# Later batches' queries transposed by VectorE in 32 by 32 blocks instead of by TensorE

## What is computed

```
q_s = exp(q - max over features); q_s /= sum over features + 1e-9
k_s = exp(k - max over tokens);   k_s /= sum over tokens + 1e-9
x = q_s @ (k_s^T @ v)                      per batch and head -> [4608, 512]
x = relu(x @ w_in)^2 @ w_out               512 -> 2048 -> 512
x = (silu(xn @ w_gate) * (xn @ w_val)) @ moe2_w_out,  xn = x / rms(x) * rms_g   512 -> 1536 -> 512
```

## Time and profile before

| | |
|---|---|
| median of 3 runs | 1659.6 us (1659.34 to 1660.26) |
| the profiled execution, its own time | 1660.84 us |
| its span in the trace | 1659.1 us |
| TensorE busy | 1642.0 us, 99% |
| VectorE, ScalarE, GpSimd busy | 1155.2, 616.8, 595.6 us |
| granted TensorE clock over the span | 0.999 of full speed |

### The profile page before, as it was taken

One profiled execution on the slowest core, in us unless ns is written; L12 is line 12 of the kernel. 1 busy time (PEld: TensorE's weight loads), 2 busy tenths in 40 slices (PEclk: granted clock), 3 DMA queues, 4 the chain that ended last, 5 costly groups with the idle time before them and its releaser, 6 DMA issues.

```text
span 1659.1 us, 27077 instructions
## 1 busy us (share of the span) xinstructions
PE 1642.0 (99%) x10246; PEld 1494.9 (90%) x10246; DVE 1155.2 (70%) x1752; ACT 616.8 (37%) x1056; POOL 595.6 (36%) x469
## 2 busy tenths in 40 slices
PE   7999999999999999999999999999999999999999
PEld 6999999999988888888888988988998989999999
DVE  6687667666667778888766565546555568877785
ACT  5544334333323333333334333323333334434442
POOL 4554324332102225342237644556455553000000
PEclk9999999999999999999999999999999999999999
DMA  7675545554653453444341323232321335443441
GB/s 260 200 247 182 172 163 184 185 175 134 213 176 84 127 172 115 123 122 124 109 158 71 105 93 112 87 127 89 108 88 65 112 124 178 153 153 121 147 140 52
DMA packets 151745, 230.10 MB, mean 139 GB/s; under 512 B 11840, under 2 KB 75840, under 8 KB 151616
## 3 DMA queue, kind: packets, MB, share of 16 engines
q1 hardware_dynamic: 151616, 228.38, 42.4%
HBM read 143.39 MB, written 84.93 MB: 138 GB/s over the span
## 4 chain that ended last, share of the span: by engine, by line
PE 93%; DVE 2%; POOL 2%; issue 1%; ACT 1%; SPq 0%; DMA 0%; DVEq 0%; ACTq 0%; POOLq 0%
PE bank L1882 16%; PE bank L1884 16%; PE bank L1883 16%; PE bank L1968 7%; PE bank L1969 7%; PE bank L1970 7%; PE bank L2057 5%; PE bank L2059 5%; PE bank L2058 5%; PE bank L1875 2%; PE bank L1855 1%; PE bank L1871 1%; PE bank L1903 1%; PE bank L1904 1%; PE bank L1905 1%
## 5 line engine op out<-in xcount | busy, mean ns | idle before, releaser
L1882 PE MATMUL bank<-TR,SW 128*128 128x512 f32 (+1 forms) x840 | 308.7, 367 | 0.3 <-DVE TR L1590 0.3
L1884 PE MATMUL bank<-TR,SW 128*128 128x512 f32 (+1 forms) x840 | 308.7, 368 | 0.0
L1883 PE MATMUL bank<-TR,SW 128*128 128x512 f32 (+1 forms) x840 | 308.6, 367 | 0.0
L1882 PE MATMUL bank<-TAR,SA 128*128 128x288 f32 x784 | 249.0, 318 | 0.1
L1883 PE MATMUL bank<-TAR,SA 128*128 128x288 f32 x784 | 231.2, 295 | 0.0
L1884 PE MATMUL bank<-TAR,SA 128*128 128x288 f32 x784 | 230.4, 294 | 0.0
L1968 PE MATMUL bank<-GH,W 128*128 128x512 f32 x576 | 224.2, 389 | 0.4 <-DVE GH L1495 0.4
L1969 PE MATMUL bank<-GH,W 128*128 128x512 f32 x576 | 224.2, 389 | 0.0
L1970 PE MATMUL bank<-GH,W 128*128 128x512 f32 x576 | 224.2, 389 | 0.0
L1172 ACT ACTIVATE GH<-g 128x512 fp32r<-128x512 f32 x144 | 91.1, 633 | 241.6 <-DVE g L1490 161.4
L2058 PE MATMUL bank<-SW,OA 128*128 128x256 f32 x630 | 178.3, 283 | 0.0
(11 more groups left out here) (178 smaller groups left out, 3306.0 us busy)
## 6 DMA issues: line engine op xcount, KB each, us to landing
h_scratch<-hb SPq DMA_DIRECT2D x128, 288.0 KB, 2.6
hst<-h_scratch SPq DMA_DIRECT2D x144, 256.0 KB, 2.7
araw<-a_scratch SPq DMA_DIRECT2D x18, 1536.0 KB, 6.8
a_scratch<-group SPq DMA_DIRECT2D x72, 256.0 KB, 2.0
xst<-xn_scratch SPq DMA_DIRECT2D x10, 1024.0 KB, 5.4
xn_scratch<-x SPq DMA_DIRECT2D x9, 1024.0 KB, 5.4
a_scratch<-group SPq DMA_DIRECT2D x48, 192.0 KB, 1.9
out<-ost SPq DMA_DIRECT2D x36, 256.0 KB, 2.0
```

Source lines behind the costliest of these rows:

```text
L1882: nc.tensor.matmul(ps[:, 0:w], w_hi[:, cc], x_hi[:, c], start=opens and c == 0, stop=False, skip_group_check=True)
L1883: nc.tensor.matmul(ps[:, 0:w], w_lo[:, cc], x_hi[:, c], start=False, stop=False, skip_group_check=True)
L1884: last = nc.tensor.matmul(ps[:, 0:w], w_hi[:, cc], x_lo[:, c], start=False, stop=c == 1, skip_group_check=True)
```

## The change

For batches 1 to 7 the host lays out the queries so that a partition holds (head, half of the features, token within a block of 32), and its row holds 18 token blocks by 32 features. A transpose of each 32 by 32 block within its 32 partitions then gives qT. Because a token's 64 features are now on two groups of 32 partitions, maxima and sums are taken over 32 features and combined: ScalarE copies each quarter's column to the neighbouring quarter (four small copies, twice per unit), and VectorE takes the maximum or the sum of both. The rounds Q0 and Q1 and their reads are gone for the later batches; one VectorE transpose (qturn) takes their place, and X0 and X1 wait for it. There is one DMA for q instead of two. Batch 0 is as before.

```diff
-UNIT_PE = [("KM", -3), ("Q0", 0), ("Q1", 1), ("KV", 2), ("X0", 6), ("X1", 7)]
-UNIT_DVE = [("qmax", -10), ("qsum", -6), ("qinv", -6), ("kmax", -9), ("readKM", -2), ("readKV", 3)]
-UNIT_ACT = [("qexp", -7), ("kexp", -1), ("readQ0", 1), ("readQ1", 2), ("readX0", 7), ("readX1", 8)]
-UNIT_POOL = [("qsub", -9), ("qnorm", -4)]
+UNIT_PE = [("KM", -3), ("KV", 2), ("X0", 6), ("X1", 7)]
+UNIT_DVE = [("qmax", -12), ("kmax", -9), ("qmax2", -9), ("qsum", -6), ("qinv", -3), ("readKM", -2), ("qturn", 0), ("readKV", 3)]
+UNIT_ACT = [("qmaxswap", -10), ("qexp", -7), ("qsumswap", -4), ("kexp", -1), ("readX0", 7), ("readX1", 8)]
+UNIT_POOL = [("qsub", -9), ("qnorm", -3)]
...
-            qn[i], at = place(f"qn{i}", at, [P, SJ, 2, D])
+            qn[i], at = place(f"qn{i}", at, [P, SB, DQ])
...
-        CONSTS, CONSTS_ALONE, CONSTS_Q = 13, 6, 2
+        CONSTS, CONSTS_ALONE, CONSTS_Q = 11, 6, 2
...
+        def swap_quarters(dst, src):
+
+            for i in range(P // DQ):
+                rows, other = slice(i * DQ, (i + 1) * DQ), slice((i ^ 1) * DQ, (i ^ 1) * DQ + DQ)
+                last = nc.scalar.activation(dst[rows, :], src[other, :], ACT.Copy)
+            return last
...
-                if unit(b, c) > KC + 2:
-                    sp.wait_ge(rnd_ready, ROUND_NO[b - (c < 2), "Q1", (c - 2) % KC])
+                if b:
+                    if unit(b, c) > KC + 2:
+                        sp.wait_ge(q_turn, unit(b, c) - KC - 2)
+                    sp.dma_start(bufs(b, c).q, qb_d[b - 1, c]).then_inc(loads(b, c)[1][0], 16)
+                    return
...
-                lambda: nc.gpsimd.memset(qn[0][TAIL:P, FULL], 0.0),
-                lambda: nc.gpsimd.memset(qn[1][TAIL:P, FULL], 0.0),
...
+                if b and what == "qsub":
+                    pool.wait_ge(q_max2, u - KC)
+                    nc.gpsimd.tensor_tensor(q, q, over_block(qmax_own[:, :]), ALU.subtract).then_inc(q_sub, 1)
+                    return
+                if b:
+                    pool.wait_ge(q_inv, u)
+                    nc.gpsimd.tensor_tensor(q, q, over_block(qscale[:, :]), ALU.mult).then_inc(q_norm, 1)
+                    return
...
+                elif what == "qmaxswap":
+                    act.wait_ge(q_max, u)
+                    swap_quarters(qmax_other, qmax_own).then_inc(q_maxswap, 1)
+                elif what == "qsumswap":
+                    act.wait_ge(q_sum, u)
+                    swap_quarters(qsum_other, qsum_own).then_inc(q_sumswap, 1)
...
+                elif what == "qmax2":
+                    dve.wait_ge(q_maxswap, u - KC)
+                    nc.vector.tensor_tensor(qmax_own[:, :], qmax_own[:, :], qmax_other[:, :], ALU.max).then_inc(q_max2, 1)
...
+                elif what == "qturn":
+                    dve.wait_ge(q_norm, u)
+                    if (b, c) != (1, 0):
+                        dve.wait_ge(rnd_ready, ROUND_NO[b - (c < 1), "X1", (c - 1) % KC])
+                    nc.vector.transpose(m.qT, m.q.rearrange("p n d -> p (n d)")).then_inc(q_turn, 1)
+                elif what == "qinv" and b:
+                    dve.wait_ge(q_sumswap, u - KC)
+                    nc.vector.scalar_tensor_tensor(qsum_own[:, :], qsum_own[:, :], EPS_SUM, qsum_other[:, :], ALU.add, ALU.add)\
+                      .then_inc(q_den, 1)
+                    dve.wait_ge(q_den, u)
+                    dve.wait_ge(q_norm, u - 1)
+                    nc.vector.reciprocal(qscale[:, :], qsum_own[:, :]).then_inc(q_inv, 1)
...
-                    wait_taken(pe, ROUND_NO[b, "Q1" if half else "Q0", c] - 1)
+                    if b:
+                        pe.wait_ge(q_turn, u - KC)
+                    else:
+                        wait_taken(pe, ROUND_NO[b, "Q1" if half else "Q0", c] - 1)
...
+    qb = q[1:].reshape(B - 1, KC, 2, SB, DQ, 2, DQ).transpose(0, 1, 2, 5, 4, 3, 6).reshape(B - 1, KC, P, SB, DQ)
```

More of the change, by code:

```diff
@@ L20 @@
 TA = S // 2
+DQ = 32
+SB = S // DQ
 FA, FB = 2048, 1536
@@ L310, with build @@
 Bufs = namedtuple("Bufs", "kT q v ekS qT bd kmax qmax")
-def build(nc, q4_d, q1_d, kT_d, k5_d, v4_d, v1_d, w1_d, s1_d, w2_d, wB_d, gv_d, out):
+def build(nc, q4_d, q1_d, qb_d, kT_d, k5_d, v4_d, v1_d, w1_d, s1_d, w2_d, wB_d, gv_d, out):
     h_d = nc.dram_tensor("h_scratch", [P, CA, B * S], F32, kind="Internal").ap()
@@ L412, in build @@
         kinv, at = place("kinv", at, [P, 1])
-        qmax, at = place("qmax", at, [P, SJ, 2])
         qden, at = place("qden", at, [P, SJ, 2])
         qinv, at = place("qinv", at, [P, SJ, 2])
+        qmax_own, at = place("qmax_own", at, [P, SB])
+        qmax_other, at = place("qmax_other", at, [P, SB])
+        qsum_own, at = place("qsum_own", at, [P, SB])
+        qsum_other, at = place("qsum_other", at, [P, SB])
+        qscale, at = place("qscale", at, [P, SB])
         HB = [[None] * H_SETS, [None] * H_SETS]
@@ L452, in build @@
         q_max, q_sub, q_exp = sem("q_max"), sem("q_sub"), sem("q_exp")
+        q_maxswap, q_max2, q_sumswap, q_turn = sem("q_maxswap"), sem("q_max2"), sem("q_sumswap"), sem("q_turn")
         q_sum, q_den, q_inv, q_norm = sem("q_sum"), sem("q_den"), sem("q_inv"), sem("q_norm")
@@ L502, in over_d, with over_block @@
             return t.rearrange("p j (h o) -> p (j h) o", o=1).to_broadcast([P, SJ * 2, D])
+        def over_block(t):
+            return t.rearrange("p (n o) -> p n o", o=1).to_broadcast([P, SB, DQ])
+        def swap_quarters(dst, src):
[3 more added lines that the diff above has]
+            return last
         def unit(b, c):
@@ L513, in bufs @@
             i = c % 2
-            return Bufs(kT[i][:, :], qn[i][:, :, :, :], vn[i][:, :, :], kt[i][:, :, :], qT[:, :], bd[:, :], kmax[:, :],
-                        qmax[:, :, :])
+            return Bufs(kT[i][:, :], qn[i][:, :, :], vn[i][:, :, :], kt[i][:, :, :], qT[:, :], bd[:, :], kmax[:, :],
+                        qmax_own[:, :])
         def loads(b, c):
@@ L521, in loads @@
             n = (b - 1) * (KC // 2) + c // 2 + 1
-            return (kT_in[c % 2], 16 * n), (q_in[c % 2], 32 * n), (v_in[c % 2], 32 * n)
+            return (kT_in[c % 2], 16 * n), (q_in[c % 2], 16 * n), (v_in[c % 2], 32 * n)
         def round_bank(n):
@@ L918, in attention @@
                 u = unit(b, c)
-                q = bufs(b, c).q.rearrange("p j h d -> p (j h) d")
+                q = bufs(b, c).q
+                if b and what == "qsub":
[6 more added lines that the diff above has]
+                    return
+                q = q.rearrange("p j h d -> p (j h) d")
                 if what == "qsub":
@@ L1416, in attention @@
                         dve.wait_ge(q_inv, u - 1)
-                    nc.vector.tensor_reduce(qden[:, :, :], m.q, axis=AX.X, op=ALU.add).then_inc(q_sum, 1)
+                    nc.vector.tensor_reduce(qsum_own[:, :] if b else qden[:, :, :], m.q, axis=AX.X, op=ALU.add).then_inc(q_sum, 1)
+                elif what == "qturn":
[10 more added lines that the diff above has]
+                    nc.vector.reciprocal(qscale[:, :], qsum_own[:, :]).then_inc(q_inv, 1)
                 elif what == "qinv":
@@ L2137 @@
     arrays = {
-        "q4": q4,
-        "q1": q1,
+        "q4": q4[0:1],
+        "q1": q1[0:1],
+        "qb": np.ascontiguousarray(qb),
         "kT": np.ascontiguousarray(k.reshape(B, KC, 2, S, D).transpose(0, 1, 2, 4, 3)).reshape(B, KC, P, S),
```

## The result

The changed kernel is slower: 1671.8 us (median of four runs, 1670.16 to 1672.06) against 1659.6 us. The ratio is 1.007, with a 95% interval from 1.0057 to 1.0082, so about 12.2 us were lost where 12.5 had been forecast as a gain.

The account below looks back on a forecast made before the run. TensorE, busy for 99% of the span, was taken as the bound. 15.2 + 1.1 - 1.9 - 1.4 - 0.5 = 12.5 us saved gave 1647.1 us against the median of 1659.6, range 1642.5 to 1653.0.

Parts of the forecast that it names:

- The added waits, in a settled batch: Settled batches: the longer chain of a unit still meets its deadlines, narrowest room 0.3 us at step 28; cost 0.
- Removed from TensorE: TensorE: Q0 and Q1 cost 0.54 us a unit, 15.2 us for 28 units, plus one wait of 1.1 us.
- Durations: VectorE and ScalarE: transpose 0.75 us, swap of four copies 0.8, maxima and sums about 0.75, combining maximum like 0.22.
- the lower bound of 0.5 us: ScalarE: a swap may take only 0.5 us if its copies overlap by 0.11 us as two reads do.
- the forecast of 1646.3: Whole kernel by the skill's ScalarE prices: a swap about 0.5 us, the two new waits 0.8 us shorter, 1646.3 us.
- The first later unit: Start, near 36 us: TensorE waits 1.9 us for ScalarE's half result behind the second swap, replacing the old 1.1.
- The first unit of batch 2: Near 103 us: the second swap lengthens the chain to X0, whose wait grows by 1.4 us.
- Rival 2: Every settled batch: late readKM and kexp delay the fourth product's copy; 0.2 to 0.3 us a unit, 1652.7 to 1655.5; chance 0.14.
- Rival 4: Each unit: ScalarE's and VectorE's in-order queues hold each other back, copies over 0.5 us; slower, 1675 us at 1 us; chance 0.05.
- Rival 1: Whole kernel: no new wait, swaps overlap and the early chain catches up; saving 16.8 us, 1642.8 us; chance 0.12.
- Rival 3: TensorE: transposes are worth only 0.08 us each, 11.2 us in all; 1651.1 us; chance 0.05.
- Rival 5: Whole kernel: nothing gained, VectorE at 80% becomes pace maker with 0.45 us a unit; about 1659.6 us; chance 0.04.

Follow-up runs that it names:

- run 3: Changed kernel without both exchanges between quarters, and with qmax, qinv and qnorm at their old steps (-10, -6, -4): 1646.64 us.
- run 5: Changed kernel with qmax2 one step earlier (-10, ahead of kmax) and qmaxswap at -11: 1660.0 us.
- run 7: Changed kernel with ScalarE's split of B22 put ahead of the swap of the second unit's maxima on the same step: 1667.67 us.
- run 12: Run 11 with one ScalarE copy of 128x18 within the partitions in place of four for each exchange of the first two units: 1652.01 us.
- run 14: Run 11 with the second unit's qmax2, qsub and kmax behind VectorE's split of B22, its sums' exchange behind ScalarE's read of X0: 1649.32 us.
- run 13: Run 11 with more tasks of the first two units moved, among them the first's qmax to -16 and the second's kmax to -7: 1660.2 us.
- run 1: Kernel before, without rounds Q0 and Q1 and their reads for batches 1 to 7 (X0 and X1 multiply zeros): 1645.21 us.
- run 4: Changed kernel with VectorE transposing only one of a unit's 18 blocks: 1671.16 us.
- run 11: Changed kernel with single tasks of the settled batches' first two units moved (qmaxswap, qmax2, qmax, qsub) and batch 1's first unit at step 12: 1656.91 us.
- run 2: Changed kernel without both exchanges between quarters, each half of the features normalised by itself: 1652.6 us.

## Why the prediction was wrong

**The step that failed** is "The added waits, in a settled batch", with its end "That is the narrowest place, and it holds by my durations: cost 0". It worked out one unit, the one at step 28, whose neighbours in the queues are h copies. The units at steps 8 and 17 have their maxima, swaps and subtractions between steps 52 and 8, where VectorE and ScalarE also split x. In the place of 0, the runs show 4.07 us a settled handover, 23.9 in all. The text read slack from busy shares (VectorE at 80%) although it also wrote that the queue is in order; which task stands ahead of which was followed at one base step of four. Its own limit, "wrong if a settled batch is over 53.2 us long", was passed by 3.6 us.

**The cost has three parts**, by runs 3, 5, 7, 12 and 14. (a) Tasks put ahead of others with earlier deadlines: the second unit's maxima, at step 5 instead of 7, stand ahead of readKM at step 6; its swap stands ahead of ScalarE's split. (b) Tasks put too far back: qmax2 behind kmax and h_22, 3.5 us after its input was there. (c) The exchange in the chain itself, 0.9 us twice. Part (c) costs little alone, since run 14 keeps it; it uses up the room that (a) and (b) need. On top of (a) and (b) comes what they set side by side: a VectorE split that begins under a GpSimd operation takes up to 1.62 us instead of 0.75 (runs 7 and 13, and the last section). How much of the 6.0 us of run 3 is this and how much is readKM behind the maxima was not separated.

**Removed from TensorE: right.** 15.2 + 1.1 stood against 14.9 measured (28 x 0.54 is 15.1, a slip of 0.1); the price of a unit (0.54) is that of the settled batches (0.55), 0.11 for each of the five transposes. At 400 us the trace of run 1 is 17.0 us ahead of that of the kernel before; what is missing in the end, 1.5 us, goes behind the first part, most of it at the wait near 1373 us (1.4 us against 0.3).

**Durations: right.** Transpose 0.77 us (0.75 taken), swap 0.90 (0.8), sum 0.75, combining maximum 0.19 (0.22). The copies of a swap show no overlap: they start 0.23 us apart at 0.216 each, so neither the lower bound of 0.5 us nor the forecast of 1646.3 that rests on such an overlap came true. That VectorE's transpose is hidden was right as well (run 4).

**The first later unit: right.** 1.9 us were worked out, TensorE waits 1.95, and for what was said: ScalarE's half result behind the second swap, which runs from 34.40 to 35.30. In the timeline, beside the earlier trace rows:

```profile
35.32 0.41 ACT L1180 ACTIVATE hb<-bank 128x288 f32<-128x288 f32 x1
35.79 0.40 PE L1955 MATMUL bank<-TAR,SA 128*128 128x288 f32 x1 [1.95 <-ACT hb L1180]
```

**The first unit of batch 2: right in kind, wrong in place and size.** A wait of 2 us before X0 near 103 was expected. There are three waits, before KV, before B22 and before X0 (beside the earlier trace rows):

```profile
98.15 0.80 PE L1904 MATMUL bank<-vn,kt 128*64 128x65 f32 x20 [1.92 <-issue]
101.14 0.40 PE L1934 MATMUL bank<-TAR,SA 128*128 128x288 f32 x1 [1.19 <-DVE TAR L1524]
105.98 0.75 PE L1927 MATMUL bank<-qT,bd 128*128 128x288 f32 x2 [0.77 <-ACT xa L1163]
```

This is the first of the handovers: two of the three are the waits of every later batch. The view was on the right spot and took it for an exception of the start.

**The rivals.** Rival 2 had the first half of the largest wait (readKM and kexp late), but let the copy for the fourth product suffer, where it is KV that waits for kexp, and priced it at 0.2 to 0.3 us for each of 28 units; it is 1.49 us at one product a batch. Rival 4 had the sign and the in-order queues, but hung them on a copy dearer than 0.5 us, which it is not (0.216), and in each unit. Its chance was 0.05, and that the time came out slower is no credit to its mechanism. A rival "the tasks moved by two steps stand ahead of the splits at each handover", worked out from the lists of steps, was missing. Rivals 1, 3 and 5 fell: there are new waits, the transposes are worth the full price, and VectorE is no pace maker (run 14 has more busy time on it in the settled stretch, 42.74 us, than the kernel after).

## What to carry to other kernels

When a change lengthens a chain that is spread over in-order queues, write out for every place of the schedule, not for one, what stands directly ahead of and behind each moved task, and compare their deadlines: busy shares do not show it. A short task in a long chain is placed by when its input is there and by what waits behind it, and the time of a copy on one engine is best filled on the other with work that has a deadline (run 14 against run 11). When a task moves, look also at what it then runs beside on another engine (run 13). When a change loses, first take the additions out one by one: here the idea was worth 15 us, the additions cost 26.6, and 22.5 of these were their places in the lists.

## What the hardware showed beside this

A VectorE operation with both inputs in SBUF is held by a GpSimd operation that is under way. Two rows of the handover of the kernel after (timeline), as an instance:

```profile
312.25 1.44 POOL L974 TENSOR_TENSOR xa<-xa 128x576 f32<-128x576 f32 x1 [1.09 <-DVE TAR L1524]
312.75 1.55 DVE L1524 TENSOR_TENSOR TAR<-TAR,TAR 128x576 fp32r<-128x576 f32 x1
```

GpSimd's sum ends at 313.69 and the split at 314.30, 0.61 us later. The next pair (the sum from 313.76 to 315.59, the split from 314.59 to 316.21) ends 0.62 us apart. Alone a split takes 0.75 us, so 0.14 us of it was done under the sum. The other way round, GpSimd's subtraction takes 1.61 us when it begins under such a split (318.92, the split beginning at 318.76 and ending at 319.51), and 1.16 alone. Reductions (0.75 us), the block transpose (0.77), and operations with an input in PSUM (0.44 us), are not longer beside GpSimd. In the kernel before the addition of epsilon (128x10, one input in SBUF) was longer beside it too, 0.47 to 0.61 us in four instances, and 0.17 otherwise. The Trainium skill (SBUF — State Buffer, sections SBUF: two separate sides and Who interferes with whom) says that VectorE with two SBUF inputs and a GpSimd operation that reads SBUF exclude each other, the first to begin holding the port for its whole length; these rows agree, but for the 0.14 us. This puts a price on a moved task that no list of steps shows: qmax, at step -12, delays the second split of the handover until GpSimd has begun its sum. The group of that split in run 13, where qmax stands at -16 (with qmax at -10, in run 3, it has the same mean):

```profile
L1528 DVE TENSOR_TENSOR TAR<-TAR,TAR 128x576 fp32r<-128x576 f32 x7 | 5.3, 752 | 0.0
```

In the kernel before it is 752 ns too. With qmax at -12 it is 1434 ns, in run 14 too. There a batch is 0.30 us late at its first two products, as in runs 2, 5, 7, 11 and 12 and in the kernel after, which have 1434 ns as well; run 3, with 752, loses nothing at them. But run 13 has 752 and loses 0.35 there, with the swap of the maxima at -12, so the split's length is not the only thing that makes them late. A kernel with run 14's order and qmax of the first unit back at -10 was not run; whether the 0.30 us would go, and how the 0.21 at KV would, stays open.
